# The two DRAM writes of a regrouping set apart in SyncE's sequence, with four direct transfers behind each

## The chip, the cores and the metric

One core of one Trainium2 chip runs the kernel. The metric is the device time of one execution in microseconds (us). Before the change it is 2680.96 us, the median of 3 runs (2680.41 to 2684.88).

## What is computed

Three stages follow one another, all in float32. The attention is

```python
kv_pool = kv.reshape(B, H // r, r, W // r, r, C).mean(axis=(2, 4))   # r = 4
k = v = kv_pool.reshape(B, -1, C) @ w_sr                             # 768 keys of 128
s = scale * (q @ k.transpose(0, 2, 1)); s = s - s.max(-1, keepdims=True)
a = np.exp(s); a /= a.sum(-1, keepdims=True) + 1e-09
x = (a @ v).reshape(B * N, C)                                        # B = 2, N = 12288, C = 128
```

and then two networks of 2048 hidden units run over the 24576 rows of x, the first with h * cos(h), the second with h / (1 + exp(-1.702 h)) between its two products.

## The kernel before

The attention fills the first 600 us or so, the two networks the rest. The change touches the attention alone.

**Chunks.** The rows of q are cut in 48 chunks of 512 (TOK), each of 4 tiles of 128 rows (SUB). TensorE (PE) makes the scores of a tile (128 x 768), VectorE (DVE) their maximum (L1259), ScalarE (ACT) the exponentials, and DVE turns them in blocks of 32 x 32 (`turned`, L1271). After such a blockwise transpose each 32 x 32 block has been turned in itself, but the blocks still sit in the partitions of their rows: block (a, f), with `a` the group of 32 rows and `f` the group of 32 keys, has to move from partitions 32a.. to partitions 32f... That move is the regrouping, and DMAs do it, one chunk at a time.

**The regrouping.** `regroup(c)` (L458 to L481) is issued by SyncE (SP), whose only work in the kernel is to wait and to issue DMAs. The four groups `a` of a chunk go two ways:

- Groups 0 and 1 (a < DIRECT = 2) go straight from SBUF to SBUF: for each of them four *direct transfers* of 32 partitions x 3072 B (L475), eight a chunk.
- Groups 2 and 3 go through DRAM: each is written by one *bounce write* of 384 KB (L469), and one *read back* of 768 KB (L479) brings both to their places. SP waits for both writes (`bounced`) before it issues the read back.

Three sets of buffers take turns (c % 3). The consumers are ACT, which rounds two thirds of `gathered` (L1057), and GpSimd (POOL), which rounds the last third (L613). Both wait until all nine transfers into `gathered` have landed (REGROUPED). PE's products with the values (L763, L765, L775) wait for them.

**SP's order.** SP's sequence is written out by hand: a loop over the 48 chunks (L524 and on). A pass holds the load of the queries of chunk c + 3 (L455), in the first 12 chunks a load of 512 KB of kv of the second batch (L449), `regroup(c)`, the save of the inverse sums (L487), and the save of the chunk's output of three chunks ago (L492). In chunks 18, 31 and 35 weights are loaded, in chunk 44 the first inputs of the networks. Every wait stops all of SP, so whatever stands behind it in the sequence is late too.

In the words below, "the chunk at 305.37" is the one whose first bounce write SP issues at 305.37 us.

Of the kernel before, what the change touches and what calls it, by code (L numbers as in the profile page):

```python
# [22 lines left out]
BLK = 32  # L23
# [17 lines left out]
def attention_and_networks(nc, q, kv, w_sr, w1_in, w1_out, w2_in, w2_out, out):  # L41
# [4 lines left out]
    KEYS = (H // R) * (W // R)  # L46
# [44 lines left out]
    GROUPS = P // BLK  # L91
# [10 lines left out]
    DIRECT = GROUPS // 2  # L102
# [68 lines left out]
    for b in range(B):  # L171
# [4 lines left out]
        for n in range(3):  # L176
            at = gathered_at[b] + n * CHUNK_BYTES
# [10 lines left out]
    for n in range(2):  # L188
        at = turned_at[1] + 2 * CHUNK_BYTES + n * 2 * 4 * TOK
# [181 lines left out]
    def flat(x):  # L371

        return x.rearrange("p k t -> p (k t)")
# [61 lines left out]
    with nc.Block() as block:  # L435

        @block.sync
        def _(sp):
# [19 lines left out]
            def regroup(c):  # L458

                b, n = c // CB, c % 3  # L460
                sp.wait_ge(turned_made, (c + 1) * SUB)
                if c >= 3:
                    sp.wait_ge(values_summed, c - 2)
                if c == CB + 1:
                    sp.wait_ge(piece_made, 4)
                dst, src = gathered[b][n], turned[b][n]
                for a in range(DIRECT, GROUPS):
                    at = slice((a - DIRECT) * KEYS, (a - DIRECT + 1) * KEYS)
                    sp.dma_start(  # L469
                        bounce[c][:, :, at].rearrange("f p x -> p f x"),  # L470
                        src[a * BLK:(a + 1) * BLK, :, :, :].rearrange("p f k t -> p f (k t)")
                    ).then_inc(bounced[n], 16)
                for a in range(DIRECT):
                    for f in range(GROUPS):
                        sp.dma_start(flat(dst[f * BLK:(f + 1) * BLK, a]),  # L475
                                     flat(src[a * BLK:(a + 1) * BLK, f])
                                     ).then_inc(regrouped[n], 16)
                sp.wait_ge(bounced[n], BOUNCED * (c // 3 + 1))
                sp.dma_start(dst[:, DIRECT:GROUPS].rearrange("p a k t -> p (a k t)"),  # L479
                             bounce[c].rearrange("f p x -> (f p) x")  # L480
                             ).then_inc(regrouped[n], 16)  # L481
# [42 lines left out]
            for c in range(CHUNKS):  # L524
                if c + 3 < CHUNKS:
                    load_queries(c + 3)
                if c < HT * SUB:
                    load_late_rows(c)
                if c == 18:
                    sp.wait_ge(part_copied, HT)  # L530
                    load_weight(0)
                    load_weight(1)
                if c == 31:
                    load_weight(2)
                if c == 35:
                    load_weight(3)
                regroup(c)
                save_inverse(c)
                if c >= 3:
                    save_x1(c - 3)  # L540
                if c == CHUNKS - 4:
                    sp.wait_ge(w_split, WEIGHT_PIECES)
                    for n in range(2):
                        sp.wait_ge(x1_saved[n], 16)
                        sp.wait_ge(inverse_saved[n], 16)
                        load_x1(n, n)
# [933 lines left out]
```

## Time and profile before

| | |
|---|---|
| median of 3 runs | 2680.96 us |
| the profiled execution, its own time | 2679.44 us |
| its span, first to last instruction | 2677.7 us |
| mean granted TensorE clock | 0.992 |
| busy share of the span: PE, POOL, DVE, ACT | 97%, 81%, 78%, 70% |
| data moved | 193.88 MB, 72 GB/s on average |
| share of SPq L475 in the chain that ended last | 7% |

The profile cuts the span in 40 slices of 67 us. In the first eight, which are the attention, the DMA engines are busy for 7 to 9 tenths of a slice, and from the tenth on for 0 or 1 tenth. Instructions of SP are not counted as busy, but the trace has their start and duration: the duration of a DMA instruction on SP is how long SP is held by issuing it, not how long the data takes. "To landing" is the time from the start of the issue to the semaphore's last step.

### The profile page before, as it was taken

How to read it: one execution, taken by the hardware profiler on the slowest of the kernel's cores; microseconds unless marked ns; L12 is line 12 of the kernel's file. 1: busy time of each engine (PE TensorE's matmuls, PEld its weight loads, DVE VectorE, ACT ScalarE, POOL GpSimd, SP SyncE). 2: the span in 40 equal slices, each digit the busy share in tenths (PEclk: the TensorE clock that was granted, in tenths of full speed). 3: DMA queues.
4: the chain of work that ended last, by engine and by line, in shares of the span. 5: the costliest groups of instructions: out<-in, count | busy, mean ns of one | idle time of the engine just before them, and what ended most of it. 6: DMA issues, size and time to landing. Idle time of an engine off the chain costs nothing.

```text
span 2677.7 us, 37678 instructions
## 1 busy us (share of the span) xinstructions
PE 2594.7 (97%) x11797; PEld 2139.9 (80%) x11797; DVE 2076.1 (78%) x2264; ACT 1876.6 (70%) x2280; POOL 2172.9 (81%) x1830
## 2 busy tenths in 40 slices
PE   8998888889999999999999999999999999999999
PEld 6777766767888888888888888888888888888887
DVE  7777777777787777777777878787877787877876
ACT  4655666667777777777777777777777777777776
POOL 2776888879888888888888888888888888888873
PEclk9999999989999999999999999999999999999999
DMA  7988888850101101000101010100101000100000
GB/s 245 296 283 283 260 265 267 276 178 9 24 12 23 23 12 24 12 24 12 24 12 24 12 24 12 24 23 12 24 12 24 12 24 12 24 12 24 12 16 12
DMA packets 191147, 193.88 MB, mean 72 GB/s; under 512 B 113457, under 2 KB 138353, under 8 KB 190065
## 3 DMA queue, kind: packets, MB, share of 16 engines
q1 hardware_dynamic: 190032, 193.03, 24.6%
q8 instruction: 30, 0.49, 0.1%
q10 hardware_dynamic: 1056, 0.13, 0.0%
q14 instruction: 29, 0.23, 0.0%
HBM read 92.34 MB, written 63.01 MB: 58 GB/s over the span
## 4 chain that ended last, share of the span: by engine, by line
PE 80%; SPq 10%; DMA 5%; DVE 1%; issue 1%; POOL 1%; ACT 1%; POOLq 0%
PE psum L691 26%; PE psum L692 26%; PE psum L693 26%; SPq L475 7%; DMA gathered<-bounce 3%; SPq L469 1%; POOL g_lo L676 1%; DMA bounce<-turned 1%; DMA bounce<-turned_last 1%; PE psum L763 1%; DVE neg_max L1259 1%; PE psum L765 1%; ACT probs_t_hi L1057 1%; DVE turned L1271 0%; SPq L479 0%
## 5 line engine op out<-in xcount | busy, mean ns | idle before, releaser
L676 POOL TENSOR_TENSOR g_lo<-g,g_hi 128x512 fp32r<-128x512 f32 x768 | 1120.0, 1459 | 67.7 <-ACT g_hi L1174 7.6
L1392 DVE TENSOR_TENSOR g_lo<-g,g_hi 128x1024 fp32r<-128x1024 f32 (+1 forms) x396 | 643.4, 1625 | 433.3 <-ACT g L1169 432.0
L1167 ACT ACTIVATE g_hi<-psum 128x1024 fp32r<-128x1024 f32 (+1 forms) x396 | 397.3, 1003 | 558.8 <-PE psum L693 558.7
L673 POOL CAST g_hi<-g 128x512 fp32r<-128x512 f32 x750 | 565.1, 753 | 229.8 <-DVE g L1383 229.8
L691 PE MATMUL psum<-x_hi,w_lo 128*128 128x512 f32 x1536 | 598.6, 390 | 1.3 <-DVE g L1383 1.3
L691 PE MATMUL psum<-g_hi,w_lo 128*128 128x512 f32 x1536 | 597.9, 389 | 0.8 <-POOL g_lo L676 0.8
L692 PE MATMUL psum<-x_lo,w_hi 128*128 128x512 f32 x1536 | 598.1, 389 | 0.0
L693 PE MATMUL psum<-x_hi,w_hi 128*128 128x512 f32 x1536 | 598.0, 389 | 0.0
L692 PE MATMUL psum<-g_lo,w_hi 128*128 128x512 f32 x1536 | 597.5, 389 | 0.0
L693 PE MATMUL psum<-g_hi,w_hi 128*128 128x512 f32 x1536 | 597.5, 389 | 0.0
L1383 DVE TENSOR_TENSOR g<-psum,g 128x512 f32<-128x512 f32 x768 | 490.0, 677 | 1.9 <-ACT g L1160 1.8
L1365 DVE SCALAR_TENSOR_TENSOR g<-turns,psum 128x1024 f32<-128x1024 int32 x384 | 462.8, 1205 | 4.3 <-ACT turns L1126 4.1
L1160 ACT ACTIVATE g<-g,half_pi 128x1024 f32<-128x1024 f32 x384 | 442.5, 1152 | 5.1 <-DVE g L1365 5.1
L1126 ACT ACTIVATE turns<-psum 128x1024 int32<-128x1024 f32 x384 | 395.1, 1029 | 3.7 <-PE psum L693 3.7
L1169 ACT ACTIVATE g<-psum 128x1024 f32<-128x1024 f32 (+1 forms) x396 | 393.9, 995 | 0.0
L691 PEld LDWEIGHTS psum<-x_hi,w_lo 128*128 128x128 f32 x1536 | 288.5, 188 | 63.4 <-DVE g L1383 2.8
L691 PEld LDWEIGHTS psum<-g_hi,w_lo 128*128 128x128 f32 x1536 | 288.4, 188 | 61.8 <-POOL g_lo L676 1.6
L693 PEld LDWEIGHTS psum<-x_hi,w_hi 128*128 128x128 f32 x1536 | 288.7, 188 | 60.1
L692 PEld LDWEIGHTS psum<-x_lo,w_hi 128*128 128x128 f32 x1536 | 288.7, 188 | 59.7
L693 PEld LDWEIGHTS psum<-g_hi,w_hi 128*128 128x128 f32 x1536 | 288.2, 188 | 60.1
L601 POOL TENSOR_TENSOR probs_t_lo<-gathered,probs_t_hi 128x1024 fp32r<-128x1024 f32 x140 | 333.3, 2404 | 3.2 <-ACT probs_t_hi L1057 0.4
L692 PEld LDWEIGHTS psum<-g_lo,w_hi 128*128 128x128 f32 x1536 | 288.2, 188 | 59.6
(87 smaller groups left out, 2493.0 us busy)
## 6 DMA issues: line engine op xcount, KB each, us to landing
gathered<-bounce SPq DMA_DIRECT2D x48, 768.0 KB, 5.4
bounce<-turned SPq DMA_DIRECT2D x64, 384.0 KB, 6.2
gathered<-turned SPq DMA_DIRECT2D x256, 96.0 KB, 2.8
bounce<-turned_last SPq DMA_DIRECT2D x32, 384.0 KB, 6.2
gathered<-turned_last SPq DMA_DIRECT2D x128, 96.0 KB, 3.1
x_dram<-x_out SPq DMA_DIRECT2D x48, 256.0 KB, 5.1
x_raw<-x_dram SPq DMA_DIRECT2D x48, 256.0 KB, 2.6
x_inv<-inverse_dram SPq DMA_DIRECT2D x48, 256.0 KB, 3.4
```

The source lines that it names most:

```text
L673: nc.gpsimd.tensor_copy(g1_hi[at][:, t], g1[at][:, t]).then_inc(g1_hi_ready, 1)
L676: nc.gpsimd.tensor_tensor(g1_lo[at][:, t], g1[at][:, t], g1_hi[at][:, t].bitcast(F32), ALU.subtract).then_inc(g1_lo_ready, 1)
L691: nc.tensor.matmul(dst, w_lo, x_hi, start=start, stop=False)
L692: nc.tensor.matmul(dst, w_hi, x_lo, start=False, stop=False)
L693: return nc.tensor.matmul(dst, w_hi, x_hi, start=False, stop=stop)
L1126: nc.scalar.activation(turns[ring(i, p)][:, :], h1[buffer1(i, p)], ACT.Copy, bias=0.25, scale=1.0 / (2 * math.pi)).then_inc(turns_ready, 1)
L1160: nc.scalar.activation(g1[ring(i, p)][:, :], g1[ring(i, p)][:, :], ACT.Sin, bias=half_pi[:, :]).then_inc(cos_ready, 1)
L1167: nc.scalar.activation(g2_hi[ring2(j, p)][:, t], h2[buffer2(j)][:, t], ACT.Silu, scale=GELU)
L1169: nc.scalar.activation(g2[ring2(j, p)][:, t], h2[buffer2(j)][:, t], ACT.Silu, scale=GELU).then_inc(g2_ready, 1)
L1365: nc.vector.scalar_tensor_tensor(g1[ring(i, p)][:, :], turns[ring(i, p)][:, :], -2 * math.pi, h1[buffer1(i, p)], ALU.mult, ALU.add).then_i ...
L1383: nc.vector.tensor_tensor(g1[ring(i, p)][:, t], h1[buffer1(i, p)][:, t], g1[ring(i, p)][:, t], ALU.mult).then_inc(g1_ready, 1)
L1392: nc.vector.tensor_tensor(g2_lo[ring2(j, p)][:, t], g2[ring2(j, p)][:, t], g2_hi[ring2(j, p)][:, t].bitcast(F32), ALU.subtract).then_inc(g ...
```

## The change

The loop over the two ways is made one: bounce write of group 2, the four direct transfers of group 0, bounce write of group 3, the four direct transfers of group 1, and then, as before, the wait for both writes and the read back.

```diff
                 dst, src = gathered[b][n], turned[b][n]
-                for a in range(DIRECT, GROUPS):
-                    at = slice((a - DIRECT) * KEYS, (a - DIRECT + 1) * KEYS)
+                for a in range(DIRECT):
+                    at, away = slice(a * KEYS, (a + 1) * KEYS), DIRECT + a
                     sp.dma_start(
                         bounce[c][:, :, at].rearrange("f p x -> p f x"),
-                        src[a * BLK:(a + 1) * BLK, :, :, :].rearrange("p f k t -> p f (k t)")
+                        src[away * BLK:(away + 1) * BLK, :, :, :].rearrange("p f k t -> p f (k t)")
                     ).then_inc(bounced[n], 16)
-                for a in range(DIRECT):
                     for f in range(GROUPS):
                         sp.dma_start(flat(dst[f * BLK:(f + 1) * BLK, a]),
                                      flat(src[a * BLK:(a + 1) * BLK, f])
                                      ).then_inc(regrouped[n], 16)
```

On SP, the pass of a chunk that still has a load of kv (`kv_all<-in_kv`), before:

```order
L455 DMA q_blocks_63<-in_q 128x4x128
L449 DMA kv_all_61<-in_kv 128x1024
L469 DMA bounce<-turned0_1_77 32x4x768 x2
L475 DMA gathered0_1_80<-turned0_1_77 32x768 x8
L479 DMA gathered0_1_80<-bounce 128x1536
L487 DMA inverse_dram<-inverse0_92 4x128
L492 DMA x1_dram<-x_out1_60 128x512
```

and the same pass with the change:

```order
L455 DMA q_blocks_63<-in_q 128x4x128
L449 DMA kv_all_61<-in_kv 128x1024
L469 DMA bounce<-turned0_1_77 32x4x768
L474 DMA gathered0_1_80<-turned0_1_77 32x768 x4
L469 DMA bounce<-turned0_1_77 32x4x768
L474 DMA gathered0_1_80<-turned0_1_77 32x768 x4
L478 DMA gathered0_1_80<-bounce 128x1536
L486 DMA inverse_dram<-inverse0_92 4x128
L491 DMA x1_dram<-x_out1_60 128x512
```

One bounce write has moved behind four direct transfers. Nothing is added or taken away, the sizes are the same, and the order on PE, DVE, ACT and POOL is unchanged. The lines behind L469 have moved up by one.

## Rows read from the trace of the kernel before

**Rows 1.** Sum and longest of SP's waits by line, 76 to 535 us.
```profile
SPq L469 <- DVE turned_last L1271: 4.4, 4, 3.1
SPq L469 <- DVE turned L1271: 4.2, 8, 0.7
SPq L492 <- ACT x_out L1064: 2.0, 6, 0.4
```

**Rows 2.** All waits, 168 to 540 us: total us, times, longest.
```profile
ACT probs_t_hi L1057 <- DMA gathered<-bounce: 91.0, 31, 8.8
POOL probs_t_hi L613 <- DMA gathered<-bounce: 77.3, 32, 8.4
```

**Rows 3.** Timeline of SP, one pass: start us, us held, what.
```profile
303.41 0.59 SPq L479 DMA_DIRECT2D gathered<-bounce  x1
304.04 0.35 SPq L487 DMA_DIRECT2D inverse_dram<-inverse  x1
304.43 0.36 SPq L492 DMA_DIRECT2D x_dram<-x_out  x1
304.84 0.42 SPq L455 DMA_DIRECT2D q_blocks<-in_q  x1
305.37 1.23 SPq L469 DMA_DIRECT2D bounce<-turned  x2
306.64 7.66 SPq L475 DMA_DIRECT2D gathered<-turned  x8
314.34 0.59 SPq L479 DMA_DIRECT2D gathered<-bounce  x1
```

**Rows 4.** Chain of waits: pieces of that pass, and one of a later pass.
```profile
306.64 1.58 SPq L475
...
308.26 2.23 SPq L475
...
310.53 0.59 SPq L475
...
355.60 1.83 SPq L475
```

**Rows 5.** Bounce writes of single chunks to landing: at 305.37, at 327.68, at 33.22.
```profile
DMA to landing us min/median/max: 6.0/6.2/6.4
DMA to landing us min/median/max: 5.0/5.4/5.8
DMA to landing us min/median/max: 4.6/5.3/5.9
```

**Rows 6.** Direct transfers to landing: the last four of 305.37; all eight of 327.68.
```profile
DMA to landing us min/median/max: 2.2/2.2/2.2
DMA to landing us min/median/max: 2.1/2.2/5.4
```

**Rows 7.** Chain of waits, the first chunk: start us, us.
```profile
33.22 0.34 SPq L469
...
33.60 0.43 SPq L469
...
34.07 1.46 SPq L475
...
35.57 1.95 SPq L475
...
37.56 0.59 SPq L475
```

**Rows 8.** Busy us by engine, then clock, DMA share, GB/s, in two stretches.
```profile
76.00:168.00 92.00, 86.31 (x496) 73.28 (x495) 66.58 (x89) 54.58 (x106) 65.75 (x33) 1.00 0.94 298
168.00:540.00 372.00, 322.08 (x1641) 263.78 (x1641) 273.46 (x368) 235.81 (x452) 292.12 (x152) 0.97 0.87 268
```

**Rows 9.** All bounce writes to landing, 76 to 168 us and 168 to 540 us.
```profile
DMA to landing us min/median/max: 5.9/6.8/8.2
DMA to landing us min/median/max: 4.8/6.1/8.1
```

**Rows 10.** Timeline of SP, a pass with a load of kv.
```profile
88.19 0.97 SPq L469 DMA_DIRECT2D bounce<-turned_last  x2
89.20 7.38 SPq L475 DMA_DIRECT2D gathered<-turned_last  x8
96.63 0.58 SPq L479 DMA_DIRECT2D gathered<-bounce  x1
```

**Rows 11.** SP's waits for the bounce writes, 43 to 76 us.
```profile
SPq L479 <- DMA bounce<-turned_last: 1.2, 1, 1.2
SPq L479 <- DMA bounce<-turned: 0.9, 2, 0.5
```

**Rows 12.** Two writes of 256 KB to DRAM into empty queues (579.8 and 590.1 us).
```profile
DMA to landing us min/median/max: 2.0/2.0/2.0
```

## The prediction

> **What bounds the kernel now.** I read the busy shares first: PE holds 97% of the span, so the networks after 600 us are PE's and the change does not reach them. The attention is another matter, and there I went to the waits. From 76 to 535 us SP waits for something in only 10.6 us out of 459 [rows 1]: it is always issuing. On the other side ACT and POOL wait 91.0 and 77.3 us for the read back, in 31 and 32 of the 33 chunks of 168 to 540 us [rows 2]. So SP's sequence sets the pace: what one pass of it takes is what a chunk takes. In the pass shown the read back is issued at 303.41 and again at 314.34 us, 10.93 us later [rows 3]. **A change of 0.1 us in every pass is 4.8 us, 0.18%, of the kernel.** 0.2% (5.4 us) is about what a measurement of this kernel can tell from no change.
>
> What is the pass spent on? The eight direct transfers hold SP for 7.66 us [rows 3]. Undisturbed one costs 0.59, and with 0.04 between them eight would take 5.0. The chain's pieces say where the rest goes: the first holds SP for 1.58 and the second for 2.23, and from the third on it is 0.59 [rows 4]. They cost what they cost because of the two bounce writes ahead. The same pair is in the first chunk, 1.46 and 1.95, where no read back and no save is in flight [rows 7]. Counted from the first bounce write's issue, the first direct transfer gets through at 306.64 + 1.58 - 305.37 = 2.85 and the second at 5.12 [rows 3, 4]; in the first chunk at 2.31 and 4.30 [rows 7]. I read this as a queue behind SP that works through one bounce write in 2.0 to 2.3 us and has room for one more DMA beside it. Direct transfers are short in it: in the chunk at 327.68 the median of all eight lands 2.2 us after its issue, as late ones of other chunks do [rows 6], so nothing is left over once the second bounce write is through.
>
> **The change, part by part.** SP's own path first, counted from the first bounce write B1 and with the durations of the chunk at 305.37. B1 is issued by 0.6; the first direct transfer takes the free place by 1.2; the second is let through when B1 has been worked off, at 2.85; the third and fourth take 0.63 each. The second bounce write, B2, is issued from 4.1 instead of from 0.6. It has the queue to itself and needs 2.2 us after its issue of 0.5 to 0.6; the fifth direct transfer takes the free place, the sixth is let through at about 6.9, and the last two end at 8.2. Before, this point was 8.97 (314.34 - 305.37). SP alone would gain 0.8 us a pass, because B1 and B2 are now worked off beside two direct transfers each instead of one after the other.
>
> Then the wait for B2. Before, it is nowhere in the waits of 76 to 535 us [rows 1], because B2 lands at about 0.6 + 6.4 = 7.0 [rows 5]: 2 us to spare. That cover goes. B2 starts 3.5 us later, so its time to landing decides. The trace has no bounce write behind four direct transfers. Bounds: 4.6, the first chunk's B1 with only two loads ahead [rows 5], and 6.1, the median of 168 to 540 us [rows 9], which holds another bounce write's 2.2 us for half of them. Far below is the 2.0 of a write of 256 KB into empty queues [rows 12], far above the worst, 8.1 [rows 9]. I take 4.6, since what B2 has ahead of it is four short transfers, of which the late ones land in 2.2: the read back is issued at 4.1 + 4.6 = 8.7, a gain of 0.25 over 8.97.
>
> One thing is added to that. In some passes a late direct transfer is held too, as the fifth of the pass at 349 us, for 1.83 instead of 0.59 [rows 4]. A wait that is there anyway swallows part of that; I put 0.05 a pass on it. So 0.3 us in each of the 36 chunks from 168 us on: **-10.8 us**.
>
> The 11 chunks with a load of kv (43 to 168 us) differ. There the DMA engines themselves are busy 94% of the time against 87% later [rows 8], and the median bounce write lands in 6.8 instead of 6.1 [rows 9]. In the pass at 88.19 the read back comes 8.44 behind B1 [rows 10]; with B2 issued 0.5 in, a landing near 7.4 leaves about half a microsecond, and in the three earliest of them SP already waits, 2.1 us in all [rows 11]. Here the four direct transfers really stand ahead of B2's data: 384 KB at the 298 GB/s of this stretch [rows 8] are 1.3 us, so B2 lands at about 9.2 and the read back is 0.8 late. SP's pause lets the engines catch up, which gives back about half. 11 x 0.4: **+4.4 us**.
>
> The wait at the read back also holds what stands behind it on SP: the save of the inverse, the save of x, the loads of q and kv, and the next bounce write. All of it moves with the read back, so it is in the terms above. Direct transfers of groups 0 and 1 land well before the read back in either order. The edit to the loop's variable and slice only builds the same DMAs and costs nothing.
>
> Sum: 2679.4 - 10.8 + 4.4 = 2673.0 against the profiled execution. The median of the runs is 1.5 us above it, so **2674.5 us** beside 2680.96.
>
> A rule speaks for a larger gain. The Trainium skill (DMA: Bandwidth & Descriptors, Anatomy of one DMA) gives a DMA issued by GpSimd a fixed cost of about 2.0 us plus bytes over 436 GB/s; an estimate from it for 384 KB would be 2.9 us. By it B2 would land at 7.0, before SP is ready, and the sum would be the whole 0.8 in the 36 chunks, 2656 us. The rows of 256 KB agree with the fixed part [rows 12], but no bounce write of this trace comes near 2.9, the quickest is 4.6 [rows 5].
>
> **The rivals.**
>
> *The wait for B2 costs more than the freed hold (slower).* The place is the wait ahead of L478, the price is what B2 needs beyond 8.97 - 4.1 = 4.9 us from its issue; from there on each 0.1 us costs 4.8. With the 5.4 of the chunk at 327.68 [rows 5] the read back comes 0.5 late in 47 passes: +24, 2705 us. For it: the engines are at 87 to 94% [rows 8], and the direct transfers ahead use the same ones. Against: most of 5.4 is another bounce write and a 256 KB load ahead. The Trainium skill (DMA: Bandwidth & Descriptors, Queues, rings and completion order) has a rule on this side: an engine takes its descriptors in ring order, and the step of the semaphore lands only after all earlier writes of that engine. B2's landing would then hold the four direct transfers' too; no row here shows it by itself.
>
> *The direct transfers need the queue as long as they hold SP (no gain at all).* Then the order makes no difference to SP's path, which ends at 8.97 as before, and only the landing is left. B2 at 8.7 to 9.0 hides behind it, the kv chunks lose their 4.4, and B2's late cases a little more: about 2683 us, within 0.2% or just outside. For it: 0.59 is longer than the 0.33 to 0.43 that a bounce write holds SP in the first chunk [rows 7]. Against: the median of 2.2 to landing [rows 6]. Or the two terms of my sum simply cancel; PE, busy 86.3 of 92 us in the first stretch [rows 8], could take nothing much there.
>
> *The full gain.* B2 lands by 8.2 and all 47 passes gain 0.8: 2643 us. PE's 94% in the first stretch forbids that much there, so 2650 at best.
>
> *It does not do what it says.* The sequences on SP show that it does; the other engines' are unchanged.
>
> **How the numbers follow.** My forecast, freed hold above added wait: 0.39 (with 0.04 of it for the full gain). Wait above hold: 0.32. Cancelled or hidden: 0.29. Near the borders the cases run into each other, and the forecast's 2674.5 is itself only 6.5 under the median; its own range is 2652 to 2675.5. For 8 in 10 the range takes the landing from about 4.2 to 5.3 us in both stretches: 2656 to 2702 us.
>
> **What would show it.** In the profile after: the second direct transfer held about 1.6 to 2.2 us, the sixth about 1 to 2, the third, fourth, seventh and eighth at 0.59; their sum below 7.66. A new wait for the bounce writes ahead of L478 in most chunks, 0.3 to 0.8 us each, more in those with kv. B2 at 4.6 us to landing. Read backs 10.6 apart from 168 us on, 0.4 more than before in the kv chunks. I am wrong if the direct transfers still hold SP 7.6 us a pass (no queue of the kind), or if B2 needs over 4.9 us (slower), or if SP no longer sets the pace.

## The result and the profile after

| | before | after |
|---|---|---|
| median | 2680.63 us (6 runs, 2678.97 to 2684.88) | 2667.24 us (6 runs, 2665.59 to 2671.96) |
| profiled execution, its own time | 2679.44 us | 2668.47 us |
| its span | 2677.7 us | 2666.7 us |

The ratio is 0.9953, 95% interval 0.994 to 0.9966: the change is faster by 13.4 us, or 0.5%. The forecast was 2674.5, faster, in a range of 2656 to 2702.

SP's waits of the changed kernel, 76 to 535 us (sum in us, times, longest), against [rows 1]:

```profile
SPq L478 <- DMA bounce<-turned: 14.7, 18, 2.4
SPq L478 <- DMA bounce<-turned_last: 10.4, 12, 1.6
SPq L469 <- DVE turned_last L1270: 3.3, 3, 2.4
SPq L469 <- DVE turned L1270: 0.7, 2, 0.5
SPq L491 <- ACT x_out L1063: 0.3, 1, 0.3
```

The new wait is there, 25.1 us in 30 chunks, where there was none. After 168 us it is 0.35 us a pass on average, in chunks 1 to 11 it is 1.6. And the kernel is faster in spite of it. The timeline of SP shows one pass (start us, us held), the counterpart of [rows 3]:

```profile
304.42 0.61 SPq L469 DMA_DIRECT2D bounce<-turned  x1
305.07 3.88 SPq L474 DMA_DIRECT2D gathered<-turned  x4
308.99 0.58 SPq L469 DMA_DIRECT2D bounce<-turned  x1
309.62 3.18 SPq L474 DMA_DIRECT2D gathered<-turned  x4
312.97 0.45 SPq L478 DMA_DIRECT2D gathered<-bounce  x1
313.47 0.34 SPq L486 DMA_DIRECT2D inverse_dram<-inverse  x1
313.86 0.37 SPq L491 DMA_DIRECT2D x_dram<-x_out  x1
314.27 0.42 SPq L455 DMA_DIRECT2D q_blocks<-in_q  x1
314.80 0.62 SPq L469 DMA_DIRECT2D bounce<-turned  x1
```

The eight direct transfers hold SP for 3.88 + 3.18 = 7.06 us instead of 7.66, and the read back is issued 8.55 us after the first bounce write instead of 8.97. The chain of waits (the sequence of work and waits that ended last, followed back) has the pieces of the same pass, the counterpart of [rows 4]:

```profile
305.07 0.60 SPq L474
...
305.72 1.96 SPq L474
...
307.73 0.59 SPq L474
...
308.36 0.59 SPq L474
...
308.99 3.96 DMA bounce<-turned
...
312.97 0.45 SPq L478
```

The first direct transfer is no longer held, the second is let through at 307.68, 3.26 us after the first write's issue (2.85 was assumed; the mean of chunks 12 to 44 is 2.87), the third and fourth go through at once. The second write lands 3.96 us after its issue, and this landing, not SP's own path, ends the chain's step. Two stretches by engine, clock and DMA share, against [rows 8] (the second ends 10 us earlier here, since the attention does):

```profile
76.00:168.00 92.00, 82.57 (x466) 70.20 (x466) 62.90 (x84) 51.86 (x100) 61.78 (x32) 0.98 0.89 286
168.00:530.00 362.00, 323.21 (x1677) 265.08 (x1676) 277.97 (x373) 239.86 (x458) 296.72 (x154) 0.98 0.90 279
```

In the first stretch the DMA engines fall from 94% to 89% busy, in the second they rise from 87% to 90%: this fits a loss with the loads of kv and a gain behind them. The first bounce writes of chunks 12 and 45 say how much. Before:

```profile
168.61 1.50 SPq L469 DMA_DIRECT2D bounce<-turned  x2
...
541.90 0.86 SPq L469 DMA_DIRECT2D bounce<-turned  x2
```

After:

```profile
173.01 0.62 SPq L469 DMA_DIRECT2D bounce<-turned  x1
...
531.83 0.38 SPq L469 DMA_DIRECT2D bounce<-turned  x1
```

Up to chunk 12 the changed kernel loses 4.4 us; in the 33 passes from there to chunk 45 it gains 373.3 - 358.8 = 14.5 us, 0.44 a pass. The span's gain is 11.0 us, the medians' 13.4.

Taken over all passes of chunks 12 to 44, the ten issues ahead of the read back hold SP 8.60 us on average before and 7.87 after, and the read back comes 9.06 and 8.67 us behind the first write. For chunks 1 to 11 it comes 8.67 us behind before and 9.49 after.

### The profile page after: what moved, and what is told of

Read it like the earlier page. It is cut to its first block, busy times and chain, and to the rows that moved or that the text cites. A ratio compares the mean times of both kernels' runs of the same rounds, so it can differ in the third digit from the quotient of the medians.

```text
span 2666.7 us, 37678 instructions
## 1 busy us (share of the span) xinstructions
PE 2589.3 (97%) x11797; PEld 2136.8 (80%) x11797; DVE 2072.3 (78%) x2264; ACT 1876.0 (70%) x2280; POOL 2172.7 (81%) x1830
## 4 chain that ended last, share of the span: by engine, by line
PE 80%; DMA 8%; SPq 8%; POOL 2%; DVE 1%; issue 1%; ACT 0%; POOLq 0%
PE psum L690 26%; PE psum L692 26%; PE psum L691 26%; SPq L474 5%; DMA bounce<-turned 4%; DMA bounce<-turned_last 2%; POOL g_lo L675 1%; DMA gathered<-bounce 1%; SPq L469 1%; SPq L478 1%; POOL probs_t_lo L600 1%; DVE neg_max L1258 0%; SPq L491 0%; SPq L455 0%; PE psum L762 0%
## 5 line engine op out<-in xcount | busy, mean ns | idle before, releaser
L672 POOL CAST g_hi<-g 128x512 fp32r<-128x512 f32 x750 | 557.5, 743 | 228.4 <-DVE g L1382 228.4
```

The costliest lines, as they stand in the source:

```text
L672: nc.gpsimd.tensor_copy(g1_hi[at][:, t], g1[at][:, t]).then_inc(g1_hi_ready, 1)
```

## The experiments

All were timed in 4 to 8 runs beside the kernel before on the same chip (its medians there: 2681.74, 2680.08 and 2678.67 us for the first four, the next four and the last four). These differ by 3 us, so medians of different groups compare no closer than that; the ratios take the difference out. The expectations were put down before the runs.

### Where the second write stands

`e1_from12` keeps the old order in the chunks with loads of kv; `e2_after2`, `e3_after1` and `e4_after3` put the second write behind 2, 1 and 3 direct transfers in all chunks:

```diff
+                ahead = 4 if c >= HT * SUB else 0    # e1; 2 in e2, 1 in e3, 3 in e4
+                bounce_write(0)
+                for m in range(DIRECT * GROUPS):
+                    a, f = divmod(m, GROUPS)
+                    if m == ahead:
+                        bounce_write(1)
+                    sp.dma_start(flat(dst[f * BLK:(f + 1) * BLK, a]), ...
```

> The first 12 chunks keep the old order (both bounce writes ahead of the eight direct transfers), the 36 others have the new one. Theory A (the change gains where a bounce write no longer holds SyncE, and loses in the chunks with a load of kv, where the second write lands later than before): the change's 13.4 us are a gain of some 14 to 18 us after 168 us and a loss of about 4.4 before it (the bounce write of chunk 12 is issued at 173.01 us instead of 168.61). Expected: that write near 168.6, the whole 4 us below the change, 2663 us. Theory B (the loss in the early chunks is caught up later, because the rest of the core has slack there): the same as the change, 2667. Theory C (the early chunks are noise): 2667 as well, with chunk 12 at 173.

> The second bounce write stands behind two direct transfers instead of four. Theory A (a queue behind SyncE that works off a bounce write in 2.0 to 2.3 us and has one more place): two direct transfers are enough to fill the time of the first write, so SyncE's own path stays at 8.1 us behind the first write, and the second write is issued 1.2 us earlier and lands 1.2 us earlier or less. The wait at the read back goes almost everywhere: after 168 us the read back at 8.1 to 8.2 instead of 8.5 (0.3 us in 36 chunks, 11 us), in the kv chunks 0.8 us less (9 us): 2650 to 2655. Rival (what holds SyncE is the amount of data in flight, so the longer the writes are apart the better): the hold comes back in part, time between the kernel before and the change, 2668 to 2675.

> The second bounce write stands behind one direct transfer. Theory A: the first direct transfer takes the free place, the second write is held until the first has been worked off (2.85 us), the next direct transfer takes the place, and the one after it is held until about 5.0: SyncE's path ends at 8.9 as in the kernel before, with the read back unwaited after 168 us: within 4 us of the kernel before, 2677 to 2683. Rival (data in flight): a little better than before, a little worse than with two.

> The second bounce write stands behind three direct transfers. Theory A: SyncE's path 8.1 as with two or four, landing 0.63 us earlier than with four: the wait after 168 us is gone in most chunks, in the kv chunks half of it stays: between e2 and the change, 2654 to 2661. Rival (data in flight): between e2 and the change as well, but with e2 above and not below the change.

The column "read back" is its issue behind the first bounce write, the mean of chunks 12 to 44; "held" the sum of the ten issues ahead of it; "chunk 12" the issue of its first write.

| direct transfers ahead of the second write | median us | ratio, 95% interval | chunk 12 | held | read back |
|---|---|---|---|---|---|
| 0 (before) | 2680.63 | | 168.61 | 8.60 | 9.06 |
| 1 (e3) | 2667.60 | 0.9953, 0.994 to 0.9967 | 168.14 | 8.29 | 8.75 |
| 2 (e2) | 2660.30 | 0.9921, 0.9908 to 0.9935 | 168.14 | 7.99 | 8.48 |
| 3 (e4) | 2660.36 | 0.9919, 0.9905 to 0.9932 | 170.00 | 7.92 | 8.55 |
| 4 (the change) | 2667.24 | 0.9953, 0.994 to 0.9966 | 173.01 | 7.87 | 8.67 |
| 4 from chunk 12 on (e1) | 2667.41 | 0.9945, 0.9931 to 0.9958 | 168.39 | 7.95 | 8.69 |

The hold falls with each direct transfer that is put between, nearly all of it with the first two; the wait for the second write grows with each. Two or three are best, 7 us better than the change (8 to 9 by the ratios, whose intervals lie apart). A pass of e2, from the chain of waits (L480 is the direct transfer there, L484 the read back), shows why:

```profile
308.64 0.63 SPq L469
...
309.31 0.55 SPq L480
...
309.90 1.55 SPq L480
...
311.49 0.74 SPq L469
...
312.27 0.51 SPq L480
...
312.82 1.49 SPq L480
...
314.35 0.61 SPq L480
```

Two holds as in the change, one after each bounce write (medians 1.50 and 1.34 us, in the change 1.51 and 1.36), but the second write goes out at +2.85 instead of +4.57 and is landed when SP is ready: in chunks 12 to 44 SP's wait ahead of the read back is 0.03 us on average instead of 0.35.

The direction came as theory A said, but e2's time missed its range of 2650 to 2655 by 5 us. The read back was to come at 8.1 to 8.2 and comes at 8.48, because SP's path was put too short: its ten issues end at 8.40 (8.28 in the change). e4, at 2660.36, is inside its range of 2654 to 2661, and as good as e2 instead of between e2 and the change. The rival, the farther apart the better, had e2 above the change and is refuted.

e3 missed, 2667.60 where 2677 to 2683 was expected. The expectation counted the last direct transfers wrongly: with one place in the queue the third is held until about 5.0 and five follow, which is 8.2 and not 8.9. Typical passes of e3 do show that (medians of the ten issues 0.63, 0.52, 1.47, 0.52, 1.51 and five of 0.6, sum 7.6 as in e2), but its mean is 0.3 higher, and the kernel 7.3 us slower than e2. The surplus is spread over the second direct transfer (mean 0.77, median 0.52) and the five late ones (mean 0.67); why stays open.

e1 is half an answer. Its chunk 12 starts at 168.39: the change's loss before 168 us is the order's, and it is gone. The profiled execution took 2663.54 us, as expected, but the median of five is 2667.41, and its interval overlaps the change's. In the profiled executions 4.2 us are still there at chunk 45 (527.62 against 531.83). That they reach the end of the kernel is not shown by the medians.

### Using the wait

`e5_fill` moves the save of the inverse sums between the last direct transfer and the wait for the bounce writes; `e7_fill2` does so with the second write behind two:

```diff
                 regroup(c)
                 save_inverse(c)
+                read_back(c)         # the wait for `bounced` and the read back, out of regroup(c)
```

> The change with the save of the inverse sums moved ahead of the wait for the bounce writes, so that SyncE does 0.39 us of its own work while the second write is under way. Theory A (in the changed kernel the read back waits 1.6 us in the kv chunks and 0.35 us after, and SyncE's sequence sets the pace): up to 0.39 us a chunk come back in the kv chunks (4 us) and some 0.2 to 0.3 in the others (9 us): 2655 to 2660. Rival (DMA engines, 90% busy, set the pace and the wait is only where it shows): no change, 2667.

> As e5, but with the second bounce write behind two direct transfers. Theory A: after two direct transfers the wait is 0.6 us in the kv chunks and 0.03 after, so there is little to fill, and the read back of the later chunks comes 0.39 us later for nothing in its latency: 4 us under e2 at most, 2656 to 2661. Rival (DMA engines set the pace): the same as e2.

Both failed: 2668.55 (0.9956, 0.9943 to 0.997) and 2666.28 (0.9948, 0.9934 to 0.9961). e5 is no better than the change, which is what its rival forecast, and e7 is 6 us worse than e2, which neither of its theories did. In e5 the read back is issued 9.17 us behind the first write instead of 8.67, which takes away all that now lies less between the read back and the next pass (1.75 us instead of 2.20). The wait does get shorter, from 0.35 to 0.14 us after 168 us, and nothing is won: what was put ahead of the read back comes back as a later read back.

`e8_act_inverse` (on e2) and `e9_before_act` (on the kernel before) take that save off SP for all but the last two chunks and let ACT issue it, with the same transfers:

```diff
-                save_inverse(c)                       # on SP
+                if s % SUB == SUB - 1 and 1 <= s // SUB <= CHUNKS - 2:
+                    save_inverse(s // SUB - 1)        # in ACT's loop over the tiles
```

> As e2 (second write behind two direct transfers), with the save of the inverse sums issued by ScalarE for all but the last two chunks: 0.39 us less in SyncE's sequence a chunk, and the same transfers. Theory A (SyncE's sequence sets the pace of the attention): 46 x 0.39 = 18 us at most, some of it lost to the wait for the second write and to held transfers: 2643 to 2652. Rival (DMA engines set the pace): within 3 us of e2, 2657 to 2663, with the 0.39 us showing up as longer holds and waits.

> The kernel before with the save of the inverse sums issued by ScalarE, as e8 did to e2: 0.39 us less of SyncE's own work a chunk, the same transfers. Theory A (in the kernel before SyncE's sequence is the pace; the change took it down to where DMA landings and engines limit as well, which is why e8 gained only 3.5 us): here the 0.39 us count in full, or nearly: 10 to 18 us faster than before, 2662 to 2670. Theory E (the DMA engines were the pace before as well, and the change gained by keeping them fuller): 0 to 5 us, 2675 to 2680, and the direct transfers are held longer by what was saved.

e8: 2656.84 us, 0.991 (0.9895 to 0.9925), 3.5 us under e2 and the fastest version that computes everything. But the two intervals overlap, and the kernel before was 1.7 us faster beside e8 than beside e2, so this step is hardly told from none. e9: 2670.93 us, 0.9972 (0.9961 to 0.9982), 7.7 us under its kernel before. 0.39 us in 46 chunks are 18 us; so in the kernel before less than half of what SP is spared reaches the end, and once the order is better a fifth or less. Both results lie between their theories (e8: 2643 to 2652 or 2657 to 2663, e9: 2662 to 2670 or 2675 to 2680). The first, second and third direct transfer of one pass of e9, from the chain of waits, are held differently from before:

```profile
300.36 0.66 SPq L475
...
301.06 2.47 SPq L475
...
303.58 0.91 SPq L475
```

With the save gone from SP's sequence, the first direct transfer is held for 0.78 us in the median instead of 1.51, the second for 2.17 instead of 2.07, the third for 0.98 instead of 0.59. In sum the hold has moved and not grown: the ten issues take 8.65 us on average in chunks 12 to 44 where they took 8.60. A pass there is 11.11 us instead of 11.31, so 0.20 of the 0.39 are gained. The other 0.19 come back mostly in longer issues of other DMAs: the save of x 0.50 instead of 0.41, the two bounce writes together 1.31 instead of 1.23, the read back 0.63 instead of 0.58. So part of what SP is spared comes back as time at its other issues. Why those get longer, and what ACT's issuing costs ACT, no run separates.

### What holds a direct transfer

`e6_wide` (on the change) gives each bounce write a DRAM side of 32 runs of 12288 B instead of 128 of 3072 B:

```diff
-                        bounce[c][:, :, at].rearrange("f p x -> p f x"),
-                        src[away * BLK:(away + 1) * BLK, :, :, :].rearrange("p f k t -> p f (k t)")
+                        bounce[c].rearrange("f p x -> (f p x)").rearrange("(h p y) -> h p y", h=DIRECT, p=BLK)[a],
+                        src[away * BLK:(away + 1) * BLK, :, :, :].rearrange("p f k t -> p (f k t)")
```

`e10_small_q` (on the change) and `e12_small_q_before` (on the kernel before) load a quarter of the queries; `e11_half_bounce` (on the kernel before) halves the bounce writes and reads the written half twice:

```diff
-                sp.dma_start(q_blocks[:, :].rearrange("p (s c) -> p s c", c=C), q_rows[c])      # e10, e12
+                sp.dma_start(q_blocks[:, 0:C], q_rows[c][:, 0])
...
-                        bounce[c][:, :, at].rearrange("f p x -> p f x"),                        # e11
+                        bounce[c][:, :, at.start // 2:at.stop // 2].rearrange("f p x -> p f x"),
-                        src[a * BLK:(a + 1) * BLK, :, :, :].rearrange("p f k t -> p f (k t)")
+                        src[a * BLK:(a + 1) * BLK, :, :, :].rearrange("p f k t -> p f (k t)")[:, :, 0:KEYS // 2]
```

> The change with each bounce write's DRAM side laid out by partition, so that a partition's four runs of 3072 B become one of 12288 B; the bytes are the same. The read back is unchanged and so fetches the probabilities in another order: the keys' regrouping is left out of what is computed, the work is the same. Theory D (what holds SyncE is worked off run by run, 128 of them in a bounce write against 32 in a direct transfer): the held second and sixth direct transfer fall from 1.5 and 1.4 us to 0.6, SyncE's path from 8.1 to 6.2 us, and the landing of the second write sets the read back, near 7.3: 2630 to 2650. Rival (worked off by bytes): the holds stay, 2665 to 2669.

> The change with the loads of queries from chunk 2 on cut to a quarter (64 KB in 128 runs of 512 B instead of 256 KB in 512); the other three tiles' queries keep what the first chunk left, so most rows' scores are of other queries. Theory F (a held transfer waits for the bounce write ahead of it, which takes a fixed 2 us to work off): the second and sixth direct transfer are held 1.5 and 1.4 us as before, only the data in front of the first write's is less: 2655 to 2664. Theory G (held by the data in flight at that time, queries among them): the hold of the second falls under 1.0 us, that of the sixth stays, and 0.5 to 0.9 us a chunk are gained: 2625 to 2645.

> The kernel before with bounce writes of half the size (128 runs of 1536 B); the read back fetches the written half twice, so its size is as before, and half of the keys' probabilities in groups 2 and 3 are replaced by others. Theory F with bytes (a bounce write is worked off in 2.1 us because of its 384 KB; e6 showed that the number of runs on the DRAM side is not it): the second direct transfer is held 1.0 us instead of 2.07, the first 0.6 to 1.0 instead of 1.5, the sequence is 1.4 to 2 us shorter a chunk: 2610 to 2640. Theory F with parts (the time goes with the number of pieces of SBUF read, 4 a partition, 128 in all): the holds stay at 1.5 and 2.1 and only the engines have less to do: 2670 to 2680.

> The kernel before with the small loads of queries of e10. Theory F (fixed time for each bounce write): the first and second direct transfer are held for 1.5 and 2.1 us as before; SyncE's path stays 8.9: 2672 to 2681. Theory G (data in flight): the holds' sum of 3.6 us falls by 0.5 us or more, 2640 to 2660.

Each of the four leaves out or misplaces part of the result (e6 and e11 mix up or drop keys' probabilities, e10 and e12 most rows' queries); they are for timing only.

| | median us | ratio, 95% interval | medians of the held direct transfers, chunks 12 to 44 |
|---|---|---|---|
| before | | | first 1.51, second 2.07 |
| e12, fewer queries | 2672.63 | 0.9975, 0.9964 to 0.9986 | first 1.49, second 2.08 |
| e11, half the write | 2612.98 | 0.9755, 0.9742 to 0.9769 | first 0.51, second 0.97 |
| the change | | | second 1.51, sixth 1.36 |
| e6, longer runs | 2668.58 | 0.9953, 0.9939 to 0.9966 | second 1.55, sixth 1.32 |
| e10, fewer queries | 2657.41 | 0.9923, 0.991 to 0.9937 | second 1.70, sixth 1.32 |

Three quarters of the queries' bytes less, and not a tenth of a microsecond less hold in the pair of e12, whose pass reads like [rows 4]:

```profile
314.74 1.56 SPq L474
...
316.35 2.17 SPq L474
...
318.56 0.59 SPq L474
```

Half the bounce write, and both holds fall by a full microsecond. In a pass of e11 the timeline of SP has the eight direct transfers in 6.09 us instead of 7.66:

```profile
305.44 1.42 SPq L469 DMA_DIRECT2D bounce<-turned  x2
306.90 6.09 SPq L475 DMA_DIRECT2D gathered<-turned  x8
313.03 0.59 SPq L479 DMA_DIRECT2D gathered<-bounce  x1
```

So the hold belongs to the bounce writes and goes with their size, not with the number of runs on the DRAM side (e6) and not with the bytes of the queries in flight (e12, and e10, where the second hold is 1.70 and not shorter). All four times fell inside the range of the theory in which the bounce write ahead holds the direct transfer. What stands ahead does matter for which transfer is held: e9 above shows it, and in chunks 1 to 11 of the kernel before, with a load of kv ahead, the first direct transfer takes 0.52 us and the next three 1.18, 1.22 and 1.01 (medians). "Room for one more" describes the passes after 168 us, not every pass.

e11 takes load off the DMA engines as well, so that its 66 us are not all the hold's: the ten issues are 8.60 - 6.73 = 1.87 us less, its passes 1.3 us shorter (10.0 instead of 11.3), and SP now has new waits, for PE ahead of L455 (8.6 us) and for DVE ahead of L488 (7.2 us).

A rival is that the DMA engines' own work is the pace. Their busy share times the length of a pass estimates that work (chunks 12 to 44): 0.87 x 11.31 = 9.8 us before, 0.90 x 10.87 = 9.8 in the change, 0.84 x 11.25 = 9.5 in e12, 0.91 x 10.0 = 9.1 in e11. The change shortens the pass with the work as it was; e12 takes about 0.4 us of work away for a pass 0.06 shorter, e11 0.7 for 1.3. The engines' work alone therefore does not set the pass. It is not free either: e12 is 6 us faster than the kernel before and e10 8 to 10 us faster than the change. In both the first bounce write's issue is 0.2 us shorter (0.43 instead of 0.62 in the median).

## Why the prediction was right

**SP sets the pace, a pass is 0.1 us for 4.8.** Right for what the change did, too strong as it was put. Where the order saved SP 0.39 us on the way to the read back (9.06 to 8.67), a pass became 0.44 shorter. But e9 and e8 saved SP 0.39 us too and got 7.7 and 3.5 us for 18. "It is always issuing" [rows 1] was the weak step: SP's held time was counted as SP's own work, and it is a wait for what is behind SP. Work taken off SP anywhere else is partly handed back in its other issues. The read backs, forecast 10.6 us apart from 10.93 in one pass, came 10.48 apart in the median of chunks 12 to 44, from 10.89 (on average 10.83, from 11.27, since a few passes are long).

**A queue with one place beside a bounce write of 2.0 to 2.3 us.** Right for the passes after 168 us, and that the hold goes with the bounce write is now shown by itself (e11). What the queue is made of is not. The forecast had the first direct transfer free, the second let through at 2.85 and the sixth at 6.9, the path ending at 8.2. In the pass shown the first is free, the second comes at 3.26, and the second group takes 3.18 us. The means of chunks 12 to 44 meet the forecast closely: 2.87, 6.94 and 8.28. The ten issues came down by 0.73 us, where the path was to gain 0.8.

**The second write lands 4.6 us after its issue.** The term that was mis-sized. It measured 3.96 in that pass, and 4.27 on average in chunks 12 to 44 (issued at 4.38, landed at 8.65). The nearest row, 4.6 of the first chunk [rows 5], had a load of kv in front, which may be why it was slower. Part of it was given back by an issue later than forecast, 4.38 and not 4.1, since the third and fourth direct transfer take 0.73 and 0.63 us on average and not 0.59. The 0.05 us for late holds is not measured by itself: what the transfers behind the held ones take beyond 0.59 was 0.49 us a pass before (six of them) and 0.26 after (four). The gain was to be 0.3 us in 36 chunks and was 0.44 in 33 passes: 14.5 us where 10.8 were forecast.

**The time.** The measured gain of 13.4 us is about twice the forecast 6.5. Of the 7.3 us between 2674.5 and 2667.24, 3.7 are the term above and 0.9 were gained behind the first bounce write of chunk 45. The other 2.7 are no mechanism: the forecast put the median 1.5 us above the profiled execution, and in the changed kernel it is 1.2 below.

**The chunks with kv lose 4.4 us.** Chunk 12 is 4.4 us later than before. As an intermediate result this is exact by luck: the read back is 0.82 us late (forecast 0.8), and a pass 0.46 us longer over 11 passes would be 5.1 us, of which 0.7 had been gained before chunk 1.

**The rivals.** The wait for the second write does cost more than the hold where the engines were 94% busy before; it takes the landing beyond 4.9 us that the rival named, and there it was 9.48 - 3.67 = 5.8. After 168 us it was not reached. That the direct transfers need the queue as long as they hold SP is refuted: then the holds could not have come down. The full gain needed a landing by 8.2; the order that comes nearest to it is e2.

**The estimate from the Trainium skill.** Its fixed cost of 2.0 us plus bytes over 436 GB/s (DMA: Bandwidth & Descriptors, Anatomy of one DMA, given for DMAs that GpSimd issues) made 2.9 us for a bounce write. The bounce writes of the changed kernel, 168 to 530 us, took at least 3.7 from issue to landing:

```profile
DMA to landing us min/median/max: 3.7/5.6/8.8
```

The measured landing decides: with 2.9 the change would have had no wait at the read back, and it has one in 30 chunks. The prediction also read the 256 KB writes of [rows 12] as agreeing with the fixed part. They don't: the same rule gives an estimated 2.6 us for them, and they took 2.0 in all.

Whether the four direct transfers ahead delay the second write at all, as one would expect from the ring order in the Trainium skill (DMA: Bandwidth & Descriptors, Queues, rings and completion order), is not shown by any run. With two fewer ahead it lands 0.86 us earlier behind the first write (7.79 instead of 8.65), though it was issued 1.49 us earlier (2.89 instead of 4.38). From its own issue it needs 4.90 us with two ahead and 4.27 with four, so standing closer behind the first bounce write costs it more than the two direct transfers that are no longer ahead give back.

## What to carry to other kernels

When an issuing engine never waits and yet issues slowly, look at the duration of each single issue: a few long ones behind large writes are a hold, and small transfers put between the large ones fill it. Put in only as many as the hold is long (here two, 7 us better than four), because each one more makes the last large write land later behind the first (7.79, 8.17 and 8.65 us with two, three and four), and someone waits for it. Work that is merely moved past such a wait (e5, e7) or off the issuing engine (e8, e9) returned much less than its duration here.

## What was not expected of the hardware

- Behind a write of 384 KB from 32 partitions to DRAM SP issues one more DMA freely and is held at the next: in the change, after 168 us, the direct transfers behind the first write take 0.52 and 1.51 us in the median. Behind a pair of such writes they take 1.51 and 2.07 instead of 0.59. Half the bytes: 0.51 and 0.97. A quarter of the runs with the same bytes: no difference (1.55 and 1.32 against 1.51 and 1.36).
- The read back, twice as large, holds nobody: the save issued right behind it takes 0.34 us. So it is not the size of just any DMA. Nor is it the direction alone: behind the save of x, 256 KB from 128 partitions to DRAM, the load of the queries takes 0.42 to 0.43 us in all 33 passes of the kernel before after 168 us, while half a bounce write, 192 KB from 32 partitions, still holds the second transfer for 0.97. That points at the 32 partitions; no run here varies them.
- 0.39 us taken off SP are worth 0.17 us a chunk in the kernel before (7.7 us over 46) and at most 0.08 in e2 (3.5 us, hardly clear of the noise).
